# Finding each slot's token by an inverse of the routing, and gathering the experts' rows directly, in a fused routing and expert part

## The reference

```python
def _moe_ref(x, w_gate, w_noise, noise, w1, w2):   # x: [3072, 320], from the recurrence
    logits = x @ w_gate
    noise_scale = np.log1p(np.exp(x @ w_noise))
    noisy_logits = logits + noise_scale * noise
    top2 = np.argpartition(-noisy_logits, 2, axis=1)[:, :2]
    ...                                            # softmax over the two: top2_w
    for e in range(8):
        for k in range(2):
            mask = top2[:, k] == e
            h = np.maximum(x[mask] @ w1[e], 0.0)   # w1[e]: [320, 1024]
            out[mask] += top2_w[mask, k, None] * (h @ w2[e])
    return out
def _moe2_ref(x, w_in, w_out):                     # [320, 2048], [2048, 320]
    h = x @ w_in
    return np.maximum(0.01 * h, h) @ w_out
```

## Time and profile before

| | us |
|---|---|
| median of 3 runs | 1602.24 |
| lowest and highest of them | 1595.39, 1615.37 |
| the profiled execution | 1609.4 |
| its span, first to last instruction | 1607.7 |
| stage A, in the span | 0 to about 616 |
| stage R | about 616 to 711 |
| stage E | about 711 to 1212 |
| stage M | about 1212 to 1607.7 |

### The profile page before, as it was taken

One profiled execution on the slowest core, in us unless ns is written; L12 is line 12 of the kernel. 1 busy time (PEld: TensorE's weight loads), 2 busy tenths in 40 slices (PEclk: granted clock), 3 DMA queues, 4 the chain that ended last, 5 costly groups with the idle time before them and its releaser, 6 DMA issues. The chain is left out here.

```text
span 1607.7 us, 40558 instructions
## 1 busy us (share of the span) xinstructions
PE 1309.5 (81%) x16814; PEld 1190.1 (74%) x16814; DVE 912.3 (57%) x1553; ACT 653.6 (41%) x1451; POOL 307.7 (19%) x254
## 2 busy tenths in 40 slices
PE   3558787787888882008999999999993999999998
PEld 3437676675767672008999999999992888888887
DVE  5869575574827004307777778777762444444533
ACT  2324343343433221206666666666651333323332
POOL 3415151322522121840000000000003110110000
PEclk9957887677878675558999999999996999999999
DMA  6984545536243217446677676776732110110000
GB/s 156 337 221 111 140 113 135 130 90 158 80 102 86 78 38 215 167 157 206 212 245 230 211 254 216 234 241 206 257 129 73 34 50 17 34 49 15 1 17 17
DMA packets 142288, 219.58 MB, mean 137 GB/s; under 512 B 60202, under 2 KB 111530, under 8 KB 138762
## 3 DMA queue, kind: packets, MB, share of 16 engines
q1 hardware_dynamic: 123183, 153.68, 32.6%
q0 software_dynamic: 9088, 36.05, 6.5%
q10 hardware_dynamic: 9891, 27.97, 6.0%
HBM read 175.33 MB, written 42.34 MB: 135 GB/s over the span
## 5 line engine op out<-in xcount | busy, mean ns | idle before, releaser
L327 DVE TENSOR_TENSOR prod<-Tl,Lt 128x1 f32<-128x1 f32 (+30 forms) x186 | 150.7, 810 | 81.9 <-DMA Lt<-lscr 75.9
L1238 DVE TENSOR_TENSOR gf<-psM,low 128x512 f32<-128x512 f32 x96 | 66.4, 691 | 182.5 <-ACT low L1276 174.1
L1276 ACT ACTIVATE low<-psM 128x512 f32<-128x512 f32 x96 | 57.5, 599 | 245.7 <-PE psM L1334 223.6
L1081 PE MATMUL psE<-w2h,hh 128*128 128x320 f32 x496 | 155.7, 314 | 0.0
L1083 PE MATMUL psE<-w2h,hl 128*128 128x320 f32 x496 | 153.3, 309 | 0.0
L1082 PE MATMUL psE<-w2l,hh 128*128 128x320 f32 x496 | 153.2, 309 | 0.0
L1066 PE MATMUL psE<-xh,w1h 128*128 128x256 f32 x496 | 141.2, 285 | 5.6 <-DVE w1l L971 5.6
L1067 PE MATMUL psE<-xl,w1h 128*128 128x256 f32 x496 | 141.2, 285 | 0.0
L1068 PE MATMUL psE<-xh,w1l 128*128 128x256 f32 x496 | 141.2, 285 | 0.0
L971 DVE TENSOR_TENSOR w2l<-w2t,w2h 128x320 fp32r<-128x320 f32 x248 | 122.0, 492 | 10.8 <-ACT w2h L966 10.8
L1313 PE MATMUL psM<-woh,gh 128*128 128x320 f32 x384 | 120.4, 313 | 5.2 <-DVE gl L971 5.0
(11 more groups left out here) (171 smaller groups left out, 3292.5 us busy)
## 6 DMA issues: line engine op xcount, KB each, us to landing
w2t<-in_w_dram SPq DMA_DIRECT2D x31, 1280.0 KB, 6.2
w1t<-in_w_dram SPq DMA_DIRECT2D x31, 1024.0 KB, 8.0
w1t<-in_w_dram SPq DMA_DIRECT2D x62, 256.0 KB, 8.6
Vd<-in_vG_dram ACTq DMA_DIRECT2D x22, 640.0 KB, 6.7
xsort<-xT POOLq DMA_DIRECT2D x1, 9920.0 KB, 50.7
xs<-xsort SPq DMA_DIRECT2D x31, 320.0 KB, 5.6
ysort<-ys POOLq DMA_DIRECT2D x31, 320.0 KB, 4.1
RV<-in_rvE_dram ACTq DMA_DIRECT2D x22, 416.0 KB
```

What stands on the lines that cost most here:

```text
L327: mark(nc.vector.tensor_tensor(prod[:, 0:t, 0:t], Tl[:, 0:t, CH - t:CH], Lt[:, t:t + 1, CH - t:CH].to_broadcast([128, t, t]), ALU.mult))
L1081: mm(o, hh[:, f, sl], w2h[:, f, :], start=(f == 0), stop=False)
```

## The change

1. **No sorted copy.** `xsort`, its filling with zeros (POOL's transfer in stage A, and the wait for it), the load of `X` and the 48 scatters are gone.
2. **An inverse instead.** After `pos`, VectorE splits each position into its low 7 bits and the rest, and writes for both copies one-hot rows of the low part (`lows`, 48 blocks of 128 columns) and rows that hold the token's number at the place of the high part (`highs`, 48 blocks of 62 columns). 48 matmuls of 62 columns, which add up in one bank, yield a table of 128 x 62: the token of each slot, and 0 where a slot is padding. VectorE copies it to `src`. `lows` and `highs` lie in the memory of `wih` and `woh`.
3. **Gathers per tile.** POOL fetches the rows of each tile straight from `xrow` by two indirect transfers of 128 rows (62 in all), at most two tiles ahead of PE's turning (`e_tr`). SP no longer loads `xs`.
4. **One block.** Routing and experts form one block (`stage_re`) without a barrier between. SP loads the first tiles' `w1` as soon as `texp` is there, ahead of `pos`. The routing's small arrays lie in the memory of `w2t`, `ys` and `xs`, so the first `w2` waits for `src`.
5. **Weights of the last stage by pieces.** In every tile with an even number (16 of 31) SP loads 128 columns of `w_in` and 128 rows of `w_out`; ACT and VectorE split them at the end of the tile's work, ahead of the copy to `ys`.
6. **`ysort` is written by SP**, two tiles later in its queue, ahead of the tile's `w2` load; the last two after the loop. `xh` and `xl` have one buffer in place of two.

The core of the diff:

```diff
-            pool.dma_start(xsort.rearrange("(n p) m -> p n m", p=128), ...)   # zeros, stage A
...
-        @block.gpsimd                                    # stage_r
-            for i in range(NT):
-                for j in range(2):
-                    pool.indirect_dma_start(out=xsort[:, :], out_offset=bass.IndirectOffsetOnAxis(ap=pos[:, j, i:i + 1], axis=0),
-                                            in_=X[:, i, :], in_offset=None).then_inc(q["r_sc"], 16)
-            pool.wait_ge(q["r_sc"], 32 * NT)
...
+        @block.gpsimd                                    # stage_re
+            pool.wait_ge(q["r_src"], 1)
+            for i in range(NTS):
+                if i >= 2:
+                    pool.wait_ge(q["e_tr"], i - 1)
+                for s in range(NS):
+                    t = NS * i + s
+                    pool.indirect_dma_start(out=xs[:, i % 2, s, :], out_offset=None, in_=xrow[:, :],
+                                            in_offset=bass.IndirectOffsetOnAxis(ap=src[:, t:t + 1], axis=0)).then_inc(gx[i % 2], 16)
...
+            for j in range(2):                           # PE, after the two matmuls on M
+                pe.wait_ge(q["r_hi"], j + 1)
+                for i in range(NT):
+                    if i % 12 == 0:
+                        pe.wait_ge(q["r_lo"], 2 * j + i // 12 + 1)
+                    m = mm(ps[3][:, 0:NHI], lows[:, j, i, :], highs[:, j, i, :], start=(j + i == 0), stop=(j * i == NT - 1))
+            m.then_inc(q["r_Q"], 1)
...
+            for j in range(2):                           # DVE
+                link(tt(highs[:, j, :, :], itl..., hif[:, j, :]..., ALU.is_equal))
+                tt(highs[:, j, :, :], highs[:, j, :, :].bitcast(F32), ids..., ALU.mult).then_inc(q["r_hi"], 1)
+                for f in (slice(0, 12), slice(12, 24)):
+                    tt(lows[:, j, f, :], i128..., lof[:, j, f]..., ALU.is_equal).then_inc(q["r_lo"], 1)
...
+            nc.vector.tensor_copy(src[:, :], ps[3][:, 0:NHI]).then_inc(q["r_src"], 1)
...
+                if p == 0:                               # DVE, in every even tile, ahead of the copy to ys
+                    dve.wait_ge(q["e_mh"], n * 2 + 1)
+                    f = bass.ds(n * 128, 128)
+                    split_lo(nc, wil[:, 0:2, f], wis[:, 0:2, :], wih[:, 0:2, f]).then_inc(q["e_ml"], 1)
+                    split_lo(nc, wil[0:64, 2, f], wis[0:64, 2, :], wih[0:64, 2, f]).then_inc(q["e_ml"], 1)
+                    dve.wait_ge(q["e_mh"], n * 2 + 2)
+                    split_lo(nc, wol[:, bass.ds(n, 1), :]..., wos[:, :], woh[:, bass.ds(n, 1), :]...).then_inc(q["e_ml"], 1)
```

More of the change, by code:

```diff
@@ L971, in split_lo, with stage_re @@
     return nc.vector.tensor_tensor(lo, src, hi.bitcast(F32), ALU.subtract)
-def stage_e(nc, st, w1, w2, xsort, ysort):
+def stage_re(nc, st, noise, w_in, w_out, w1, w2, xrow, ysort):
     ctx = ExitStack()
@@ L989, in stage_e @@
         ps = [ctx.enter_context(nc.psum_tensor(f"psE{i}", [128, 512], F32)) for i in range(8)]
-        ident, texp = st["ident"], st["texp"]
+        LG, ident, triu = st["LG"], st["ident"], st["triu"]
+        gate, pos, texp = st["gate"], st["pos"], st["texp"]
+        wih, wil, woh, wol = (st[n] for n in ("wih", "wil", "woh", "wol"))
         NF, NS = F1 // 128, TS // 128
+        NSL, NHI = NT * 128 // TS, NTS * TS // 128
         w1t = sb("w1t", [128, 2, 3, F1])
@@ new lines, in stage_re @@
+        small = carve(w2t[:, :, :].rearrange("p f m -> p (f m)"))
+        nz, az, ex, nl = (small(NT, E) for _ in range(4))
+        top, idf = small(NT, 8), small(NT, 8)
+        pk = small(2, E, NT)
+        dif, e2, den = (small(NT) for _ in range(3))
+        ids, i128 = small(NT), small(128)
+        lof, hif, posf = (small(2, NT) for _ in range(3))
+        iexp, prev, cnt, ntile, endt, base = (small(E) for _ in range(6))
+        isl, gt = small(NSL), small(E, NSL)
+        idx, posl, posh = small(NT, 8).bitcast(U32), small(2, NT).bitcast(U32), small(2, NT).bitcast(U32)
@@ L1001, in stage_e @@
+        small = carve(ys[:, :, :, :].rearrange("p a b m -> p (a b m)"))
+        M, tot, run, off, pf = (small(E, NT) for _ in range(5))
+        small = carve(xs[:, :, :, :].rearrange("p a b m -> p (a b m)"))
+        oh = small(2, E, NT)
+        one, itl = small(E * NT), small(NHI)
+        ge, tef = small(NTS, E)[0:1], small(NTS)[0:1]
         ld = [sem("e_ld0"), sem("e_ld1")]
+        gx = [sem("e_gx0"), sem("e_gx1")]
         wr = [sem("e_wr0"), sem("e_wr1")]
-        names = "e_ld2 e_z e_tr e_xh e_xl e_w1h e_w1l e_w2h e_w2l e_mm1 e_hh e_hl e_mm2 e_yA e_yV".split()
+        names = ("r_nz r_wt r_io r_az r_ex r_dif r_e2 r_M r_PR r_dve r_tx r_lo r_hi r_src r_Q "
+                 "e_ld2 e_z e_tr e_xh e_xl e_w1h e_w1l e_w2h e_w2l e_mm1 e_hh e_hl e_mm2 e_yA e_yV e_mh e_ml e_mz").split()
@@ new lines, in _ @@
+            flat = "p e i -> p (e i)"
+            stt(az, LG[:, :, E:], -1.0, LG[:, :, E:], ALU.mult, ALU.max).then_inc(q["r_az"], 1)
+            link(nc.vector.memset(one, 1.0))
+            link(nc.vector.memset(prev[:, 0:1], 0.0))
+            dve.wait_ge(q["r_ex"], 2)
+            dve.wait_ge(q["r_nz"], 16)
+            link(stt(nl, LG[:, :, E:], 0.0, az, ALU.max, ALU.add))
+            link(tt(nl, nl, nz, ALU.mult))
+            link(tt(nl, nl, LG[:, :, 0:E], ALU.add))
+            for i in range(NT):
+                last = nc.vector.max(top[:, i, :], nl[:, i, :])
@@ new lines, in _ @@
+            link(last)
+            for i in range(NT):
+                last = nc.vector.max_index(idx[:, i, :], top[:, i, :], nl[:, i, :])
+            link(last)
+            link(nc.vector.tensor_copy(idf, idx))
+            dve.wait_ge(q["r_io"], 5)
+            for j in range(2):
+                last = tt(oh[:, j, :, :], iexp.rearrange("p (e o) -> p e o", o=1).to_broadcast([128, E, NT]),
+                          idf[:, :, j:j + 1].rearrange("p i o -> p o i").to_broadcast([128, E, NT]), ALU.is_equal)
@@ new lines, in _ @@
+            link(last)
+            tt(M, oh[:, 0, :, :], oh[:, 1, :, :], ALU.add).then_inc(q["r_M"], 1)
+            tt(dif, top[:, :, 1], top[:, :, 0], ALU.subtract).then_inc(q["r_dif"], 1)
+            dve.wait_ge(q["r_PR"], 1)
+            link(nc.vector.tensor_copy(tot.rearrange(flat), ps[5][:, 0:E * NT]))
+            link(nc.vector.tensor_tensor_scan(run.rearrange(flat), one, tot.rearrange(flat), 0.0, ALU.mult, ALU.add))
+            link(nc.vector.tensor_copy(prev[:, 1:E], run[:, 0:E - 1, NT - 1]))
@@ new lines, in _ @@
+            tt(off, run, tot, ALU.subtract)
+            link(tt(base, endt, ntile, ALU.subtract))
+            nc.vector.tensor_reduce(tef, ge, AX.X, ALU.add)
+            link(stt(base, base, float(TS), prev, ALU.mult, ALU.subtract))
+            ts(tef, tef, float(E - 1), None, ALU.min)
+            link(tt(off, off, base.rearrange("p (e o) -> p e o", o=1).to_broadcast([128, E, NT]), ALU.add))
+            nc.vector.tensor_copy(texp[:, :], tef).then_inc(q["r_tx"], 1)
+            dve.wait_ge(q["r_PR"], 2)
@@ new lines, in _ @@
+            link(tt(pf.rearrange(flat), ps[4][:, 0:E * NT], off.rearrange(flat), ALU.add))
+            for j in range(2):
+                last = tt(pk[:, j, :, :], oh[:, j, :, :], pf, ALU.mult)
+            link(last)
+            for j in range(2):
+                last = nc.vector.tensor_reduce(posf[:, j, :], pk[:, j, :, :].rearrange("p e i -> p i e"), AX.X, ALU.add)
+            link(last)
+            link(nc.vector.tensor_copy(pos[:, :, :], posf))
+            nc.vector.tensor_single_scalar(posl, pos[:, :, :], 127, ALU.bitwise_and)
@@ L1378, in program @@
             st[n] = sb(n, [128, F2 // 128, DM], F32R)
-        stage_r(nc, st, noise, w_in, w_out, xrow, xsort)
-        stage_e(nc, st, w1, w2, xsort, ysort)
+        stage_re(nc, st, noise, w_in, w_out, w1, w2, xrow, ysort)
         stage_m(nc, st, ysort, out)
```

328 lines of the change are left out of this document (128 added, 200 removed).

## The result

| | before | changed |
|---|---|---|
| median, us | 1598.82 (4 runs) | 1530.89 (4 runs) |
| lowest to highest | 1595.26 to 1615.37 | 1521.31 to 1535.49 |
| the profiled execution's span | 1607.7 | 1531.2 |

The account below looks back on a forecast made before the run. The path from `pos` to stage E's first matmul (91.7 us), then PE in stage E, were taken as the bound. Terms -63.9 and -1 gave -65 us: 1602.2 to 1537 us, own range 1521 to 1552, 8 in 10 within 1521 to 1560.

Parts of the forecast that it names:

- The bound: Between `pos` and tile 0's first matmul: all 91.7 us are on the path, and saving there moves all of stage E forward.
- Up to `pos`: Routing's chain on VectorE before the inverse: a few steps moved, `pos` ready at 635.8 in place of 636.2 us.
- The inverse: From `pos` to `src`: eight wide VectorE operations 14.0 us, PE's last 24 small matmuls 5.3, copy 0.3; done at 654.4 us.
- The first gathers: From `src` to the first matmul: issue 1.26, landing 2.9, VectorE's hold-up 2.0, turning and splitting 3.4 us; start at 664.0.
- Work that comes into stage E: Splits added in 16 tiles, some 1.0 us on ACT and 1.2 on VectorE, fit in idle time and cost nothing.
- The ends: Hand-over to stage M with SP writing `ysort`: -1 us (0 to -2); zero fill's removal in stage A: 0 (0 to -10).
- the dearer inverse: Rival, 8%, shared with dearer first gathers: wide operations at double price (+14 us) and the full stall (+3), 1554 us.
- a full stall beside VectorE: First gathers' issue held up by VectorE's `w1` splits: upper end 5.1 us against 2.0 taken; +3 in an 8% rival.
- A longer stage E on VectorE: Rival, 12%: each gather keeps VectorE from its memory for 0.96 us, stage E 25 us longer, 1562 us.
- POOL falling behind: Rival, 3%: gathers set stage E's pace, tiles lengthen from 7.7 us a gather; at 10 us the time is 1681 us.

## Why the prediction was right

The 1530.9 us lie 6 us below the forecast of 1537, inside the range, and came about by the mechanism that was named. By its own steps:

- **The bound.** It said that the 91.7 us from `pos` to the first matmul are all path. Right: 24 scatters fewer gave 33.2 us, 48 more gave 59.2, and in both the whole of stage E moved by it. The forecast of 63.9 us saved there was measured as 61.7.
- **Up to `pos`.** Forecast 0.4 us less, measured 0.9.
- **The inverse.** Forecast 18.6 us from `pos` to `src`, measured 18.2 (629.07 to 647.23). A wide operation took 1.71 us where 1.73 and 1.78 were taken from the broadcast product of stage M, and PE's 24 small matmuls took 5.30 where 5.3 had been worked out from the pitch of matmuls four times as wide. So between 62 and 256 columns their number does not set that pitch; that the load of the 128 x 128 block sets it, as the text argued, was not tested. PE stood idle for 11.8 + 1.4 + 9.6 = 22.7 us between the ones matmul and the first turn, not for some 30: the text had not taken off its own small matmuls.
- **The first gathers: a term mis-sized.** Forecast 9.6 us from `src` to the first matmul, measured 12.7. The hold-up by VectorE was right in kind and in sum (2.0 forecast; 0.9 + 0.8 measured, 0.2 left when VectorE was quiet). The landing was wrong: 2.88 us came from stage M, where nothing else is being loaded, but here SP starts `w2` and the next `w1` at the same moment. The text counted that `w2` had time to land and did not ask what its traffic does to the gathers. Putting the weights behind gave 3.1 us.
- **Work that comes into stage E.** Forecast free, measured free. The idle time left is 0.87 us, not 0.5, and even 1.6 us more cost nothing.
- **The ends: a second term mis-sized.** Forecast -1, measured -3.6. Issue and landing, which the text named, give 0.9; the other 2.7 lie between the landing and POOL's next gather, and their cause is open. The zero fill was forecast free, and nothing speaks against it.

The parts sum to -61.7 - 0.6 - 3.6 = -65.9 us against the -65 forecast. That it came so close is in part luck: the dearer landing and the cheaper hand-over, two misses of about 3 us each, cancelled. That the medians differ by 68 and the two first traces by 76 is stages A and M, whose scatter no step of the change explains. A slip of 1 us stands in the range: the lower end adds up to 1520, not 1521.

Of the rivals, the dearer inverse is out by its 18.2 us; the first gathers were dearer, but by the loads and not by a full stall beside VectorE. A longer stage E on VectorE is out: it did not slow down beside POOL, even with five gathers a tile. POOL falling behind is out as well: a gather took 1.84 us at most, and 7.7 would have been needed. What the splits do to the first gathers is measured: beside them (1.2 us each) the two took twice their time, and without them 1.12 and 0.95. The other 60 took 0.95 us in the median though VectorE was busy for 376 of 472 us, so it isn't every instruction of VectorE's that holds a gather up. The Trainium skill ("SBUF — State Buffer", "SBUF: two separate sides") states that VectorE can hold the port pair that it shares with POOL for a whole instruction, in a 2-port mode or, against a POOL instruction that reads SBUF, with two inputs in SBUF; the prediction left these conditions out. The splits of `w1` have two inputs in SBUF, and the slow gathers agree with it. The delay does not decide the kernel, since POOL works two tiles ahead.

## What to carry to other kernels

A chain of small indirect transfers costs its count times the issue, here 1.26 us each where nothing held them up, and it is worth a good deal of arithmetic to turn it into something that can be issued tile by tile beside other work. When the price of a transfer is taken from a stage, look at what else is on the DMA engines there and at the new place: 2.8 MB asked for in the same 3 us took a gather's landing from 3.7 to 6.9 us. Where whole times scatter by 1%, differences of a few us are settled by durations between two events of the trace; how far such a duration repeats has to be read from several executions first (0.5 us for the routing here, 17 for stage A).

## What the runs showed of the hardware that was not expected

- An indirect gather landed 6.9 us after its start beside 2.8 MB of loads and VectorE's splits, 3.7 without the loads, and 2.9 without either.
- Gathers and scatters of 128 rows, 0.96 us to issue alone, took 1.15 to 1.97 us beside VectorE's splits of 1.2 us, and up to 6.10 beside longer ones; VectorE's splits kept their 1.222 us.
- POOL's next transfer after a write of its own and a barrier started 3.7 and 6.5 us after that write's landing, and 1.1 us where POOL had been waiting at the barrier for 54 us. The cause is open.
- fp32r matmuls of 62 columns run at the same pitch (0.22 us at the low clock) as those of 256.
- Stage A took between 600.0 and 617.2 us in seven executions of the same code.
